# Attention loads freed from the store of their slot, and the first four weight pieces moved to the end of the attention, in a fused attention, expert and MLP kernel

## Time and profile before

| | |
|---|---|
| median of 3 runs | 472.85 us (472.2 to 477.99) |
| the profiled execution | 475.02 us, of which the span is 473.3 |
| mean granted TensorE clock | 0.961 |
| PE busy | 430.1 us, 91% of the span |
| DVE busy | 285.4 us, 60% |
| ACT busy | 218.3 us, 46% |
| POOL busy | 111.8 us, 24% |
| attention, first PE work to last output | about 9 to 94 us |
| routing and first gather | about 94 to 117 us |
| experts and MLP | about 117 to 466 us |

### The profile page before, as it was taken

The page is one execution under the profiler, slowest core; times in us unless marked ns, Lnnn a source line. Parts: engine busy times, 40 slices in busy tenths (PEclk is TensorE's granted clock), DMA queues, the critical chain, the costliest instruction groups (busy, mean ns, idle before and its releaser), DMA issues.

```text
span 473.3 us, 8560 instructions
## 1 busy us (share of the span) xinstructions
PE 430.1 (91%) x2922; PEld 404.2 (85%) x2923; DVE 285.4 (60%) x494; ACT 218.3 (46%) x382; POOL 111.8 (24%) x110
## 2 busy tenths in 40 slices
PE   3997988823999999999999999999999999999993
PEld 3997987812989999999999798998989989898892
DVE  8885776684577767667766564545645355553431
ACT  3454344511455646646645544444444444444320
POOL 6856567618720120220000000000300000200003
PEclk9998899965899999999999999999999999999997
DMA  8964765805595465465455342322523223400001
GB/s 207 280 242 135 245 197 178 291 17 181 178 367 178 166 223 195 164 228 191 145 201 194 133 134 66 116 86 75 192 67 126 74 80 119 135 0 0 1 0 66
DMA packets 20989, 69.50 MB, mean 147 GB/s; under 512 B 3352, under 2 KB 9769, under 8 KB 20960
## 3 DMA queue, kind: packets, MB, share of 16 engines
q1 hardware_dynamic: 18656, 64.40, 41.7%
q0 software_dynamic: 2304, 4.73, 2.9%
HBM read 64.39 MB, written 7.08 MB: 151 GB/s over the span
## 4 chain that ended last, share of the span: by engine, by line
PE 67%; DMA 10%; DVE 7%; issue 6%; ACT 3%; SPq 2%; POOL 2%; DVEq 1%; POOLq 0%; ACTq 0%
PE bank L478 31%; PE bank L497 21%; PE bank L487 10%; DMA attention_out<-x_sb 8%; ACT whi L616 2%; DMA xg<-attention_out,gidx 1%; DVE wlo L909 1%; DMA vx<-in_vx 1%; DVE hlo L918 1%; PE bank L428 1%; PE bank L469 1%; DVE xslo L913 1%; SPq L282 1%; SPq L283 1%; SPq L284 1%
## 5 line engine op out<-in xcount | busy, mean ns | idle before, releaser
L909 DVE TENSOR_TENSOR wlo<-raw,whi 128x1536 fp32r<-128x1536 f32 x56 | 98.4, 1758 | 94.7 <-ACT whi L616 94.6
L616 ACT ACTIVATE whi<-raw 128x1536 fp32r<-128x1536 f32 x56 | 83.2, 1488 | 84.3 <-PE bank L497 47.1
L398 POOL DMA_INDIRECT out<-osb,oidx x12 | 13.0, 1082 | 245.0 <-ACT osb L731 242.6
L497 PE MATMUL bank<-whi,hhi 128*128 128x384 f32 x192 | 64.9, 338 | 0.5 <-DVE hlo L928 0.5
L497 PE MATMUL bank<-wlo,hhi 128*128 128x384 f32 x192 | 64.8, 338 | 0.0
L497 PE MATMUL bank<-whi,hlo 128*128 128x384 f32 x192 | 64.8, 338 | 0.0
L478 PE MATMUL bank<-xshi,whi 128*128 128x240 f32 x192 | 55.2, 287 | 3.4 <-DVE xslo L913 1.8
L478 PE MATMUL bank<-yhi,whi 128*128 (+1 forms) x144 | 57.1, 396 | 0.0
L478 PE MATMUL bank<-yhi,wlo 128*128 (+1 forms) x144 | 57.0, 396 | 0.0
L478 PE MATMUL bank<-ylo,whi 128*128 (+1 forms) x144 | 56.6, 393 | 0.0
L487 PE MATMUL bank<-hhi,whi 128*128 128x240 f32 x192 | 54.7, 285 | 0.0
(11 more groups left out here) (155 smaller groups left out, 832.0 us busy)
## 6 DMA issues: line engine op xcount, KB each, us to landing
raw<-in_wts SPq DMA_DIRECT2D x56, 768.0 KB, 4.3
feat<-in_feat SPq DMA_DIRECT2D x12, 448.0 KB, 4.0
rk<-in_rk SPq DMA_DIRECT2D x12, 384.0 KB, 4.6
vx<-in_vx SPq DMA_DIRECT2D x12, 224.0 KB, 5.2
vT<-in_vT SPq DMA_DIRECT2D x12, 192.0 KB, 4.0
attention_out<-x_sb SPq DMA_DIRECT2D x12, 192.0 KB, 5.2
out<-rl SPq DMA_DIRECT2D x12, 192.0 KB, 3.2
xg<-attention_out,gidx POOLq DMA_INDIRECT x24, 3.9
```

What stands on the lines that cost most here:

```text
L398: nc.gpsimd.indirect_dma_start(out=out[:, :], out_offset=bass.IndirectOffsetOnAxis(ap=oidx[:, t:t + 1], axis=0), in_=osb[:, t, :], in_offs ...
L497: mm = pe.matmul(ps_o[tt][:, 0:DM], x[:, par, ft, tt * P:(tt + 1) * P], w[:, r, cols], start=(v == 0 and ft == 0 and step == 0), stop=(v = ...
L616: return nc.scalar.activation(dst, src, ACT.Copy)
L909: v.tensor_tensor(wlo[:, r, :], raw[:, r, :], whi[:, r, :].bitcast(F32), ALU.subtract).then_inc(w_lo, 1)
```

## The change

Four things are done. (1) In rounds 1 and 2 the SP queue no longer waits for the store before it issues the slot's loads. (2) DVE waits instead, ahead of its write to `x_sb[u]`, for the store of the chunk four places back; so that the wait also holds in round 0, four small writes (to a tile that is otherwise unused this early) add 16 to each `x_stored[u]`, and POOL's final count rises by 16. (3) Weight pieces 0 and 1 are no longer loaded behind round 0's inputs, nor 2 and 3 ahead of the last four stores. Piece 0 is now issued behind the store of chunk 8, and (4) pieces 1, 2 and 3 behind the store of chunk 11, the last one.

```
@@ SP
             load_chunk(0, u)
             ...
-            load_weights(0, 0)
-            load_weights(1, 1)
             with sp.Fori(1, NC_ // 2) as i:
                 for u in range(SLOTS):
                     sp.wait_ge(x_ready, 4 * (i - 1) + u + 2)
                     store_x(i - 1, u)
-                    sp.wait_ge(x_stored[u], 16 * i)
                     load_chunk(i, u)
-            load_weights(2, 2)
-            load_weights(3, 3)
             for u in range(SLOTS):
                 sp.wait_ge(x_ready, NT - SLOTS + u + 2)
                 store_x(NC_ // 2 - 1, u)
+                if u == 0:
+                    load_weights(0, 0)
+            for r in range(1, RING):
+                load_weights(r, r)
             for r in range(RING):
                 sp.wait_ge(w_lo, r + 1)
                 load_weights(RING + r, r)
@@ POOL
             for u in range(SLOTS):
-                pool.wait_ge(x_stored[u], 16 * (NC_ // 2))
+                pool.wait_ge(x_stored[u], 16 * (NC_ // 2 + 1))
@@ DVE, before the attention's loop
+            for u in range(SLOTS):
+                v.memset(r12["drop"][:, u:u + 1], 0.0).then_inc(x_stored[u], 16)
@@ DVE, in the loop, between cv (L798) and x_sb (L801)
+                    dve.wait_ge(x_stored[u], 16 * (i + 1))
                     dve.wait_ge(y_done, n + 1)
```

## The result

The changed kernel takes **470.79 us** in the median of 20 runs (467.48 to 475.43), the kernel before 475.38 in the median of 20 (472.2 to 478.74). The ratio is 0.990, with a 95% interval of 0.9875 to 0.9926: faster by 4.6 us, or 1.0%, where 11.0 us was forecast. Two later comparisons of the same two kernels gave 0.9899 (0.987 to 0.9928) and 0.9867 (0.9805 to 0.9929). The 472.85 us on which the forecast was put was the median of three runs; that of 20 is 2.5 us higher.

What follows compares the result with a forecast made beforehand. SP's store-and-load loop was taken to bound attention from chunk 4 on; 11.58 less 0.4 (DVE beside POOL) and 0.2 (DVE's added instruction) gave 11.0 us, so 472.85 - 11.0 = 461.9 us, range 459.3 to 466.

Steps and rivals of the forecast that it cites:

- SP's loop of 6.9 us: Attention: SP's store, its landing and four load issues cost 6.9 us a chunk, whatever the engines do.
- The most there is to win is 11.58 us.: Attention: with PE never held, at 5.94 us a chunk, its last output group starts at 81.91 instead of 93.49.
- DVE and POOL side by side: Attention: one DVE and POOL meeting a chunk is about free; 0.05 us in each of 8 chunks, 0.4 in all.
- Rival 2: Attention: DVE and POOL meet twice a chunk, 2 to 5 us lost; chance 0.16 together with a mild DMA bound.
- taken as 0: Behind the attention all keeps its distances; the clock's return may shift by plus or minus 1 us, counted as 0.
- Loads in time: Attention: chunk 4's `feat` arrives before 30, with 2 to 5 us of slack; later chunks are asked for 18 us ahead.
- DMA not the bound: Attention: a chunk's 1.475 MB takes 4.8 us of DMA; even 6.4 us would lose only about 1 us.
- DVE's new wait free: Attention: `x_sb` waits for a store issued 23.8 us earlier, longest landing 11.21; the instruction costs 0 to 0.4 us in all.
- The weights: Late weight pieces, landed at 92 to 95, cost nothing behind the attention; the first gather loses 0 to 1 us, taken as 0.
- 94, the mark that the prediction set for being wrong: Behind the attention: the prediction is wrong if ACT's high part of weight piece 1 ends behind 94 us.
- If `cv` and `ru` grow to a mean over 1 us.: Attention: a sign that the prediction is wrong, DVE's `cv` and `ru` averaging over 1 us beside POOL.
- Rival 3: Attention: PE pauses over about 1.6 us a chunk lower the clock; 16 us slower, 489 us; chance 0.03.

Runs made afterwards that it cites:

- e1: The kernel before with only SP's wait for the store moved to DVE, weight pieces loaded as before: 470.44 us, ratio 0.9901.
- e5: The changed kernel with POOL held at the start until DVE's `Tr` is built, and in each chunk until an earlier `x_sb` is written: 468.62 us, ratio 0.9851.
- f1: The changed kernel again, nothing edited, in the last rounds: 469.42 us, ratio 0.9867 to the kernel before.
- f3: The changed kernel with POOL held in phase in each chunk, not at the start, and weight pieces loaded as before: 469.47 us, ratio 0.987.
- e7: The changed kernel with POOL held at the start and in each chunk, and weight pieces loaded as before: 466.71 us, ratio 0.9841.
- e6: The changed kernel with POOL's four products replaced by writes of constants, but for one column in two; only attention read: chunks 1 to 10 took 60.06 us.

## Why the prediction was wrong

The direction and the mechanism were right: SP's loop was the bound of the attention, and without its wait the stage runs at nearly PE's pace. The size was wrong: 11.0 us forecast, 4.6 measured, and 470.79 lies outside of 459.3 to 466. By its steps:

- *What bounds the kernel; SP's loop of 6.9 us.* Right. The wait is gone and the chunks are shorter, and e1 shows that this part is the whole effect.
- *"The most there is to win is 11.58 us."* **This step failed first.** It took PE's times from one execution. Chunks 1 to 10 and the stretch to routing took 80.88 us there, but 79.73 and 76.06 in the two other profiles, 78.9 in the mean: 2.0 us of the gain were a draw of that execution, a good part of it the chunk of 9.40 us at the low clock. Its total time, 475.02, lies at the median of 20 runs and gave no sign of it.
- *DVE and POOL side by side: "about free", 0.4 us.* **The mis-sized term.** The floor is 60.06 + 9.84 = 69.9 us. The sum forecast the same (80.88 - 11.0), by luck: the 0.6 us that it took off stand for the 0.7 of DVE's two loop turns, which it left out. The changed kernel took 72.5 in the mean: the meetings cost 2.6 us, not 0.4. The working assumed one meeting a chunk, of at most one POOL operation, and took the start of chunk 4 at 34.84 as proof that it is free. That was none: the `cv` of the earlier trace rows began at 33.70, PE needs what follows from it only inside chunk 4, and that chunk was held by its loads. e5 shows what the working only assumed. What it missed is that a DVE operation that comes in the midst of POOL's row can wait for two or three of them (2.82 us for `cv`, 3.17 for `ru`). Rival 2 had the size, 2 to 5 us, and too small a chance, but not the mechanism: it priced two short meetings in every chunk, and the loss is mostly one or two long ones in all. What the Trainium skill's page "SBUF — State Buffer" says in "Who interferes with whom", that whoever comes later blocks until the first has finished, is borne out only in part by the rows of chunk 1: `cv` (24.85) didn't get its turn when the operation that it met had ended (25.27), but two later (27.19). What decides how many it waits for stays open: in f1 a `cv` that also began in POOL's second product waited for one more only (1.86).
- *All else "taken as 0".* It came to +1.7 us: start and chunk 0 +0.7, the stretch to the experts +0.2, experts and MLP +0.9. The start is chance between 6.9 and 8.9 us in both kernels; the last is one profile's pause, and whether the change has a part in that stays open.
- Together: 11.0 - 2.0 - 2.6 - 1.7 = 4.7.
- *Loads in time, DMA not the bound, DVE's new wait free.* Right. In no profile of the changed kernel did PE wait on a DMA behind chunk 0, or `x_sb` on a store, though the DMA's share in 20 to 40 was 0.85 in the first and 1.04 in the second: it was full there and still ahead of PE.
- *The weights.* Right in the time: no cost, e1 and the changed kernel being alike. ACT's high part of piece 1 ended at 96.5 in the changed kernel's first profile, later than 94, the mark that the prediction set for being wrong, and even that didn't delay DVE, whose routing came later too.
- *"If `cv` and `ru` grow to a mean over 1 us."* `ru` did, in three of the four profiles (1.05 to 1.11, `cv` 0.93 in the first). But in e5, at the floor, `ru` had a mean of 1.12: the mean is the wrong sign, and the longest one the right one.
- *Rival 3, decided at a pause of about 1.6 us.* No profile shows such a border: the clock fell behind 1.09 and 0.47 us in f3 and stayed at 1.00 behind 1.33 and 0.47 in another.
- *The median.* It was the median of three runs; that of 20 is 2.5 us higher, which makes 461.9 too low by as much by itself.

The best medians are those of e5 and e7 (ratios 0.9851 and 0.9841); they are faster than before for certain, and faster than the changed kernel perhaps.

## What to carry to other kernels

When a wait that paced the loads is taken away, look at what the pauses had kept apart: an engine that now has its inputs at other times can run beside operations that it didn't meet before, and another that shares something with it may wait through several of its operations. Fixing the phase of the engine with time to spare (a wait on the other one's progress) restored PE's pace in full in two profiles of six and in part in most of the others; the runs don't show a gain of it over the changed kernel. And a limit read from one execution is a draw like its total: read the stretch that is to shrink in more than one profile before its excess is counted as a gain.

## What the runs showed of the hardware

A DVE operation with two inputs in SBUF can wait through several POOL operations that follow each other closely: `cv` took 2.82 us through the rest of one and two whole ones (24.85 to 27.67), `ru` 3.17 in another profile, against 0.63 and 0.55. With POOL writing only, both stayed at their shortest in all 12 chunks. DVE's copy `Tr`, with one input, took 1.37 us instead of 0.43 beside POOL's products at the start, and 0.90 beside a POOL fill that only writes (e6), so it isn't only two-input operations that wait. DVE's reduction `csum`, also with one input, took 0.55 us in every chunk of every profile.
